# A fused attention and MoE kernel: all four banks of y copied by ScalarE at a tile's end

## The chip, the cores and the metric

The kernel runs on one core of a Trainium2 chip. The time is the device time of one execution in microseconds (us), the median of three runs. Lower is better. The engines are TensorE (PE; PEld is its weight load), VectorE (DVE), ScalarE (ACT), GpSimd (POOL) and SyncE (SP), and they run side by side, ordered by semaphores alone.

## The reference

```python
def _attn_ref(q, k, v, tau):
    qn = q / (np.linalg.norm(q, axis=1, keepdims=True) + 1e-06)
    kn = k / (np.linalg.norm(k, axis=1, keepdims=True) + 1e-06)
    s = kn.transpose(0, 2, 1) @ qn / tau
    s = s - s.max(-1, keepdims=True)
    a = np.exp(s)
    a /= a.sum(-1, keepdims=True) + 1e-09
    return (v @ a).astype(np.float32)

def _moe_ref(x, w_in, w_out, alpha):
    h = x @ w_in
    g = np.maximum(h, 0.0) + alpha * np.minimum(h, 0.0)
    return (g @ w_out).astype(np.float32)
```

q, k and v are 2 x 6016 x 256 in float32, w_in is 256 x 2048 and w_out is 2048 x 256. The attention is over channels, so its matrix a is 256 x 256 for each of the two batches. Its output, as 12032 tokens of 256, goes through the two products with the slope between them.

## The kernel before, in words

For each batch the kernel makes the matrix a, folds it into w_in (the product is called M), and then computes M on v for tiles of tokens. A tile T is two halves of 512 tokens (448 in the last tile of a batch), and there are 12 tiles, six for each batch. The hidden dimension of a tile is worked in 8 groups, so G = 8T + jp runs over 96 groups.

In each group the up-product is done for two blocks of hidden channels and two halves of tokens, with seven block products where eight would be the plain way: sums of blocks of M and of v are multiplied, and the results are combined in the PSUM banks X (`x_ps`), Y (`p_ps`) and Z (`z_ps`). `up` does one block product in three matmuls (high times high, high times low, low times high parts). ScalarE takes X to `h` four times in a group (`take_x`, L747), VectorE adds the banks Y and Z (`add_part`, L1003) and applies the slope (`slope`, L1011), ScalarE rounds `h` to `g_hi` (`split_g_hi`, L757), and VectorE makes `g_lo` from the rest (`split_g_lo`, L1045). `down(G, k)` then multiplies g by w_out in six matmuls (L538) for each of four blocks k, and it is issued one group later than the up-products that it belongs to.

The output of a tile collects in four PSUM banks, `y_ps[t][oc]`, with t the half of tokens and oc the half of output channels. After group 8T + 7's downs, which run among the ups of group 8T + 8, the banks are copied to `y_stage` and stored. Then the next tile may begin to write the same banks: `down(8T + 8, 0)`, issued within group 8T + 9, writes the banks of t = 0, and `down(8T + 8, 1)` those of t = 1. Each waits for the copies of its two banks. There are 11 such boundaries between tiles. At the end of the last tile other code (L876) copies the banks, all on ScalarE.

Before the change ScalarE copies three banks at a boundary: [0][0] at the end of its work for group 8T + 8, and the two of t = 1 in the next group, before and after a `split_g_hi`. VectorE copies [0][1] in `take_y_dve` at the end of its own work for group 8T + 8, ahead of two `split_g_lo`. The order on each engine is the order in which the code issues; nothing reorders it.

Of the kernel before, what the change touches and what calls it, by code (L numbers as in the profile page):

```python
# [5 lines left out]
def build(nc, qk, qk_t, v_t, w_in, w_out, small, y_t):  # L6
# [9 lines left out]
    CC = C // P  # L16
# [4 lines left out]
    FJ = F // P  # L21
# [6 lines left out]
    ALL = B * TILES  # L28
    JP = FJ // 2
    GROUPS = ALL * JP  # L30

    def half_width(T):
        t = T % TILES
        return HALF if t < TILES - 1 else (N - 2 * HALF * (TILES - 1)) // 2

    def first_token(T):
        return T // TILES * N + T % TILES * 2 * HALF
# [41 lines left out]
    with ctx:  # L79
        def sb(name, shape, dt=fp32):  # L80
            return ctx.enter_context(nc.sbuf_tensor(name, shape, dt))

        def pb(name, shape):
            return ctx.enter_context(nc.psum_tensor(name, shape, fp32))

        def sem(name):
            return ctx.enter_context(nc.semaphore(name))
# [56 lines left out]
        y_stage = sb("y_stage", [P, 2, CC, HALF])  # L144
# [14 lines left out]
        y_ps = [[pb(f"y_ps{t}{oc}", [P, HALF]) for oc in range(CC)] for t in range(2)]  # L159
# [22 lines left out]
        y_stored = [sem(f"y_stored{n}") for n in range(2)]  # L182
# [26 lines left out]
        w_lo_ready = sem("w_lo_ready")  # L209
# [21 lines left out]
        down_done = sem("down_done")  # L231
        bank_done = sem("bank_done")
        y_copied = sem("y_copied")
        y_copied_dve = sem("y_copied_dve")
        dve_step = sem("dve_step")


# [38 lines left out]
        def _(sp):  # L276
# [26 lines left out]
            def load_v(T):  # L303
                b, t = T // TILES, T % TILES
                H = half_width(T)
                if T > 0:
# [3 lines left out]
                for kc in range(CC):  # L310
                    sp.dma_start(v_stage[:, 2 * kc:2 * kc + 2, 0:H],
                                 v_t[b, kc, :, n0:n0 + 2 * H].rearrange("p (t h) -> p t h", t=2)
                                 ).then_inc(v_loaded, 16)
# [14 lines left out]
            def store(T, t):  # L328
                H = half_width(T)
                n0 = first_token(T) + t * H  # L330
                sp.wait_ge(y_copied, 3 * T + 1 + 2 * t)
                if t == 0:
                    sp.wait_ge(y_copied_dve, T + 1)
                sp.dma_start(y_v[:, :, n0:n0 + H], y_stage[:, t, :, 0:H]).then_inc(y_stored[t], 16)

            for i in range(RING):
# [52 lines left out]
            H = half_width(ALL - 1)  # L389
            n0 = first_token(ALL - 1)  # L390
            for n in range(2 * CC - 1):
                t, oc = n // CC, n % CC
                sp.wait_ge(y_copied, 3 * (ALL - 1) + n + 1)
                sp.dma_start(y_v[:, oc, n0 + t * H:n0 + (t + 1) * H], y_stage[:, t, oc, 0:H]
                             ).then_inc(y_stored[t], 16)

            sp.wait_ge(y_copied, 3 * (ALL - 1) + 2 * CC)
            sp.dma_start(y_v[:, CC - 1, n0 + H:n0 + H + H // 2], y_stage[:, 1, CC - 1, 0:H // 2]
                         ).then_inc(y_stored[1], 16)
            sp.wait_ge(y_stored[0], 16 * (ALL - 1 + CC))  # L400
# [32 lines left out]
        def _(pe):  # L433
# [84 lines left out]
            def down(G, k):  # L518
                T, jp = G // JP, G % JP
                H = half_width(T)  # L520
                f, t = BLOCKS[k]
                j = 2 * jp + f
                pe.wait_ge(g_lo_ready, 4 * G + k + 1)
                if jp == 0 and k < 2:
                    if T > 0:

                        pe.wait_ge(y_copied, 3 * (T - 1) + 1 + 2 * t)
                        if t == 0:
                            pe.wait_ge(y_copied_dve, T)
                    else:  # L530

                        pe.wait_ge(m_out, CC * (t + 1))
                if T == 0 and k == 0:
                    pe.wait_ge(w_lo_ready, 2 * jp + 2)
                for oc in range(CC):
                    ws = slice(oc * P, (oc + 1) * P)
                    for w_part, g_part in ((w_hi, g_hi), (w_hi, g_lo), (w_lo, g_hi)):
                        product = nc.tensor.matmul(  # L538
                            y_ps[t][oc][:, 0:H], w_part[:, j, ws], g_part[:, k, 0:H],
                            start=jp == 0 and k < 2 and w_part is w_hi and g_part is g_hi,  # L540
                            stop=jp == JP - 1 and k >= 2 and w_part is w_lo, skip_group_check=True)
                product.then_inc(down_done, 1)
# [37 lines left out]
            for G in range(GROUPS):  # L580
                T, jp = G // JP, G % JP
# [64 lines left out]
        def _(act):  # L646
# [38 lines left out]
            def load_exp():  # L685
                nc.scalar.activation(warm[:, :], ones[:, 0:1], ACT.Exp)
# [72 lines left out]
            def take_y(T, t, oc):  # L759
                H = half_width(T)  # L760
                act.wait_ge(down_done, 4 * (JP * T + JP - 1) + 3 + t)
                if T == 0:

                    act.wait_ge(w_lo_ready, FJ)
                else:
                    act.wait_ge(y_stored[t], 16 * T)
                nc.scalar.copy(y_stage[:, t, oc, 0:H], y_ps[t][oc][:, 0:H]).then_inc(y_copied, 1)
# [39 lines left out]
            for G in range(GROUPS):  # L807
                T, jp = G // JP, G % JP
                take_x(G, 0, 0)
                if jp == 1 and T > 0:  # L810
                    take_y(T - 1, 1, 0)
                if G > 0:
                    split_g_hi(G - 1, 3)
                if jp == 1 and T > 0:
                    take_y(T - 1, 1, 1)
                if G == ROOT_G:
                    take_root(1)
                if G == EXP_G:
                    exponentials(1)
                if G == 0:  # L820
                    split_m_hi(0, 1)
                if G == 2:
                    split_m_hi(0, 3)
                if G in M_SPLIT:
                    split_m_hi(*M_SPLIT[G])
                if T + 1 < ALL:
                    for op in (V_ACT_FIRST if T == 0 else V_ACT).get(jp, ()):
                        if T == 0 and op == B11:

                            act.wait_ge(qk1_summed, len(LATE_STEPS))  # L830
                        split_v_hi(T + 1, op)
                take_x(G, 1, 3)
                if G == 0:
                    take_m(0, 2)
                if G in PAIR_AT:
                    split_pair_hi(PAIR_AT[G])
                if G == BROADCAST_G:
                    copy_rq(1)
                if G == MOVE_G:
                    split_at_hi(1)  # L840
                if G in M_AT:
                    take_m(*M_AT[G])
                take_x(G, 2, 1)
                split_g_hi(G, 0)
                if G == 0:
                    split_m_hi(0, 2)
                for n in SQ_AT.get(G, ())[:1]:
                    square_rows(n)
                take_x(G, 3, 2)
                if G == 0:  # L850
                    take_m(0, 3)
                for k in (1, 2) if G < GROUPS - 1 else (2, 1):
                    split_g_hi(G, k)
                if jp == 0 and T > 0:
                    take_y(T - 1, 0, 0)
                for n in SQ_AT.get(G, ())[1:]:
                    square_rows(n)
                if G == SUMS_G:
                    nc.scalar.activation(warm[:, :], ones[:, 0:1], ACT.Sqrt)
                if G == ROOT_G:  # L860
                    load_exp()
                if G in SLICE_AT:
                    split_slice_hi(SLICE_AT[G])
                for j in W_AT.get(G, ()):
                    split_w_hi(j)
            split_g_hi(GROUPS - 1, 3)
            H = half_width(ALL - 1)
            for n in range(2 * CC):
                t, oc = n // CC, n % CC
# [4 lines left out]
                for part in range(parts):  # L874
                    ns = slice(part * H // parts, (part + 1) * H // parts)
                    nc.scalar.copy(y_stage[:, t, oc, ns], y_ps[t][oc][:, ns]).then_inc(y_copied, 1)  # L876
            act.wait_ge(y_copied, 3 * (ALL - 1) + 2 * CC + 1)
            n0 = first_token(ALL - 1) + H
            nc.scalar.dma_start(y_v[:, CC - 1, n0 + H // 2:n0 + H], y_stage[:, 1, CC - 1, H // 2:H]
                                ).then_inc(y_stored[1], 16)  # L880
# [2 lines left out]
        def _(dve):  # L883
# [145 lines left out]
                nc.vector.tensor_tensor(slice_lo[:, :, :], w_slice[:, n % RAW_RING, :, :],  # L1029
                                        slice_hi[:, :, :].bitcast(fp32), ALU.subtract).then_inc(slice_lo_ready, 1)  # L1030

            def take_y_dve(T):
                H = half_width(T)
                dve.wait_ge(down_done, 4 * (JP * T + JP - 1) + 3)
                if T == 0:

                    dve.wait_ge(w_lo_ready, FJ)
                else:
                    dve.wait_ge(y_stored[0], 16 * T)
                nc.vector.tensor_copy(y_stage[:, 0, 1, 0:H], y_ps[0][1][:, 0:H]).then_inc(y_copied_dve, 1)  # L1040

            def split_g_lo(G, k):
                H = half_width(G // JP)
                dve.wait_ge(g_hi_ready, 4 * G + (k + 1 if G < GROUPS - 1 else LAST_ORDER.index(k) + 1))
# [54 lines left out]
            for G in range(GROUPS):  # L1099
                T, jp = G // JP, G % JP  # L1100
# [46 lines left out]
                    split_g_lo(G, 2)  # L1147
                dve.wait_ge(c12_done, G + 1)
                slope(G, 3)
                if jp == 0 and T > 0:  # L1150
                    take_y_dve(T - 1)
                for k in (1, 2) if G < GROUPS - 1 else (1,):
                    split_g_lo(G, k)
                if G == ROOT_G:
# [42 lines left out]
```

## Time and profile before

| | us |
|---|---|
| median of three runs (1076.49 to 1076.99) | 1076.69 |
| time of the profiled execution | 1076.63 |
| its span, first to last instruction | 1074.8 |
| PE busy | 1070.9 |
| PEld busy | 906.2 |
| DVE busy | 847.0 |
| ACT busy | 654.6 |
| POOL busy | 40.4 |

The span and the profiled execution's time differ by what lies around the instructions. Busy time is the union of an engine's instructions; matmuls overlap in it, since one starts before the one ahead has ended. The granted clock of TensorE was 1.0 over the execution.

### The profile page before, as it was taken

How to read it: one execution, taken by the hardware profiler on the slowest of the kernel's cores; microseconds unless marked ns; L12 is line 12 of the kernel's file. 1: busy time of each engine (PE TensorE's matmuls, PEld its weight loads, DVE VectorE, ACT ScalarE, POOL GpSimd, SP SyncE). 2: the span in 40 equal slices, each digit the busy share in tenths (PEclk: the TensorE clock that was granted, in tenths of full speed). 3: DMA queues.
4: the chain of work that ended last, by engine and by line, in shares of the span. 5: the costliest groups of instructions: out<-in, count | busy, mean ns of one | idle time of the engine just before them, and what ended most of it. 6: DMA issues, size and time to landing. Idle time of an engine off the chain costs nothing.

```text
span 1074.8 us, 13902 instructions
## 1 busy us (share of the span) xinstructions
PE 1070.9 (100%) x4995; PEld 906.2 (84%) x4995; DVE 847.0 (79%) x1349; ACT 654.6 (61%) x1100; POOL 40.4 (4%) x54
## 2 busy tenths in 40 slices
PE   9999999999999999999999999999999999999998
PEld 7888888888888888888998888888888888888898
DVE  6999987877877777787798887777777777787776
ACT  6676677667766555655666655555555555555544
POOL 0000000000000000000000000000000000000000
PEclk9999999999999999999999999999999999999999
DMA  9621154455453102103212101201202202200101
GB/s 382 284 88 50 40 158 127 138 160 150 134 162 99 30 13 54 45 9 79 69 30 73 50 11 49 59 8 52 59 1 59 59 0 54 57 1 10 40 1 35
DMA packets 30837, 80.07 MB, mean 74 GB/s; under 512 B 2992, under 2 KB 9264, under 8 KB 29232
## 3 DMA queue, kind: packets, MB, share of 16 engines
q1 hardware_dynamic: 24288, 67.80, 18.1%
q0 software_dynamic: 6336, 11.28, 6.8%
q8 instruction: 39, 0.64, 0.2%
q14 instruction: 30, 0.25, 0.1%
q10 hardware_dynamic: 144, 0.11, 0.0%
HBM read 64.04 MB, written 12.32 MB: 71 GB/s over the span
## 4 chain that ended last, share of the span: by engine, by line
PE 100%; ACT 0%; issue 0%; POOL 0%; POOLq 0%
PE y_ps L538 47%; PE x_ps L512 24%; PE z_ps L512 12%; PE p_ps L512 6%; PE x_ps L444 4%; PE s_ps L464 3%; PE p_ps L498 2%; PE s_ps L444 1%; PE y_ps L498 1%; PE y_ps L553 0%; PE z_ps L440 0%; PE p_ps L486 0%; PE p_ps L473 0%; PE p_ps L479 0%; ACT y_stage L876 0%; PE s_ps L435 0%
## 5 line engine op out<-in xcount | busy, mean ns | idle before, releaser
L538 PE MATMUL y_ps<-g_hi,w_hi 128*128 128x512 f32 (+1 forms) x760 | 293.1, 386 | 0.0
L538 PE MATMUL y_ps<-g_hi,w_lo 128*128 128x512 f32 (+1 forms) x760 | 292.9, 385 | 0.0
L538 PE MATMUL y_ps<-g_lo,w_hi 128*128 128x512 f32 (+1 forms) x760 | 292.9, 385 | 0.0
L757 ACT CAST g_hi<-h 128x512 fp32r<-128x512 f32 (+1 forms) x384 | 234.0, 610 | 78.6 <-DVE h L1011 69.3
L1011 DVE SCALAR_TENSOR_TENSOR h<-h,small_sb 128x512 f32<-128x512 f32 (+1 forms) x384 | 273.7, 733 | 0.0
L1003 DVE SCALAR_TENSOR_TENSOR h<-z_ps,sigma_neg,h 128x512 f32<-128x512 f32 (+1 forms) x192 | 141.7, 738 | 148.0 <-ACT h L747 147.6
L1045 DVE TENSOR_TENSOR g_lo<-h,g_hi 128x512 fp32r<-128x512 f32 (+1 forms) x384 | 249.9, 670 | 0.8 <-ACT g_hi L757 0.5
L747 ACT ACTIVATE h<-x_ps,sigma_neg 128x512 f32<-128x512 f32 (+1 forms) x192 | 130.7, 681 | 175.2 <-PE x_ps L512 165.1
L747 ACT ACTIVATE h<-x_ps,sigma 128x512 f32<-128x512 f32 (+1 forms) x192 | 130.6, 680 | 124.8 <-PE x_ps L512 120.2
L538 PEld LDWEIGHTS y_ps<-g_hi,w_hi 128*128 128x128 f32 x760 | 142.7, 188 | 27.3 <-issue 0.3
L538 PEld LDWEIGHTS y_ps<-g_hi,w_lo 128*128 128x128 f32 x760 | 142.7, 188 | 27.0
L538 PEld LDWEIGHTS y_ps<-g_lo,w_hi 128*128 128x128 f32 x760 | 142.7, 188 | 26.6
L512 PE MATMUL x_ps<-v_hi,m_hi 128*128 128x512 f32 (+1 forms) x384 | 148.8, 388 | 0.0
L512 PE MATMUL x_ps<-v_lo,m_hi 128*128 128x512 f32 (+1 forms) x384 | 148.1, 386 | 0.0
L512 PE MATMUL x_ps<-v_hi,m_lo 128*128 128x512 f32 (+1 forms) x384 | 148.0, 385 | 0.0
L1003 DVE SCALAR_TENSOR_TENSOR h<-p_ps,sigma,h 128x512 f32<-128x512 f32 (+1 forms) x96 | 70.8, 738 | 42.2 <-ACT h L747 42.2
L512 PEld LDWEIGHTS x_ps<-v_hi,m_hi 128*128 128x128 f32 x384 | 72.1, 188 | 14.4 <-ACT h L747 0.9
L512 PEld LDWEIGHTS x_ps<-v_hi,m_lo 128*128 128x128 f32 x384 | 72.1, 188 | 13.6
L512 PEld LDWEIGHTS x_ps<-v_lo,m_hi 128*128 128x128 f32 x384 | 72.1, 188 | 12.9
L512 PE MATMUL z_ps<-v_hi,m_hi 128*128 128x512 f32 (+1 forms) x192 | 74.3, 387 | 0.0
L512 PE MATMUL z_ps<-v_lo,m_hi 128*128 128x512 f32 (+1 forms) x192 | 74.0, 385 | 0.0
L512 PE MATMUL z_ps<-v_hi,m_lo 128*128 128x512 f32 (+1 forms) x192 | 73.9, 385 | 0.0
(129 smaller groups left out, 1009.4 us busy)
## 6 DMA issues: line engine op xcount, KB each, us to landing
rows_t<-qk_t SPq DMA_DIRECT2D x32, 376.0 KB, 4.0
stage<-qk SPq DMA_DIRECT2D x10, 1024.0 KB, 13.3
v_stage<-v_t SPq DMA_DIRECT2D x20, 512.0 KB, 4.6
y_t<-y_stage SPq DMA_DIRECT2D x20, 512.0 KB, 2.8
pair<-qk SPq DMA_DIRECT2D x19, 512.0 KB, 3.7
v_stage<-v_t POOLq DMA_DIRECT2D x27, 256.0 KB, 4.1
scratch<-w_in SPq DMA_DIRECT2D x12, 256.0 KB, 2.8
v_stage<-v_stage POOLq DMA_DIRECT2D x9, 256.0 KB, 3.3
```

Of the source, the lines that this page charges most:

```text
L444: product = nc.tensor.matmul(s_ps[b][:, kc * C:(kc + 1) * C], rows[:, C + kc * P:C + (kc + 1) * P], rows[:, 0:C], start=False, stop=last, ...
L464: product = nc.tensor.matmul(S[:, kc * C:(kc + 1) * C], k_part[:, i, ks], q_part[:, i, 0:C], start=False, stop=n == PAIRS - 1 and i == 1 a ...
L498: product = nc.tensor.matmul(bank[:, kc * 2 * P:(kc + 1) * 2 * P], a_part[:, qc, kc * P:(kc + 1) * P], w_part[:, qc, :], start=a_part is a ...
L512: product = nc.tensor.matmul(bank[:, 0:H], m_part[:, jp, a, :], v_part[T % 2][:, t, 0:H], start=start and m_part is m_hi and v_part is v_h ...
L538: product = nc.tensor.matmul(y_ps[t][oc][:, 0:H], w_part[:, j, ws], g_part[:, k, 0:H], start=jp == 0 and k < 2 and w_part is w_hi and g_pa ...
L747: nc.scalar.mul(h[:, k, 0:H], X[:, 0:H], side(k)[:, j:j + 1]).then_inc(x_copied, 1)
L757: nc.scalar.copy(g_hi[:, k, 0:H], h[:, k, 0:H]).then_inc(g_hi_ready, 1)
L1003: return nc.vector.scalar_tensor_tensor(out=h[:, k, 0:H], in0=bank[:, 0:H], scalar=side(k)[:, j:j + 1], in1=h[:, k, 0:H], op0=ALU.mult, op ...
L1011: nc.vector.scalar_tensor_tensor(out=h[:, k, 0:H], in0=h[:, k, 0:H], scalar=alpha_sb[:, j:j + 1], in1=h[:, k, 0:H], op0=ALU.mult, op1=ALU. ...
L1045: nc.vector.tensor_tensor(g_lo[:, k, 0:H], h[:, k, 0:H], g_hi[:, k, 0:H].bitcast(fp32), ALU.subtract).then_inc(g_lo_ready, 1)
```

## The change

ScalarE gets a fourth copy, of bank [0][1], right behind that of bank [0][0]. `take_y_dve` and its semaphore `y_copied_dve` go. `y_copied` now counts four copies for each tile, and the waits of SP (stores) and of PE (`down` of the next tile) count accordingly.

```diff
@@ store
-                sp.wait_ge(y_copied, 3 * T + 1 + 2 * t)
-                if t == 0:
-                    sp.wait_ge(y_copied_dve, T + 1)
+                sp.wait_ge(y_copied, 4 * T + CC * (t + 1))
@@ down
-                        pe.wait_ge(y_copied, 3 * (T - 1) + 1 + 2 * t)
-                        if t == 0:
-                            pe.wait_ge(y_copied_dve, T)
+                        pe.wait_ge(y_copied, 4 * (T - 1) + CC * (t + 1))
@@ block.scalar
                 if jp == 0 and T > 0:
                     take_y(T - 1, 0, 0)
+                    take_y(T - 1, 0, 1)
...
@@ block.vector
-            def take_y_dve(T):
-                H = half_width(T)
-                dve.wait_ge(down_done, 4 * (JP * T + JP - 1) + 3)
-                if T == 0:
-
-                    dve.wait_ge(w_lo_ready, FJ)
-                else:
-                    dve.wait_ge(y_stored[0], 16 * T)
-                nc.vector.tensor_copy(y_stage[:, 0, 1, 0:H], y_ps[0][1][:, 0:H]).then_inc(y_copied_dve, 1)
...
                 slope(G, 3)
-                if jp == 0 and T > 0:
-                    take_y_dve(T - 1)
                 for k in (1, 2) if G < GROUPS - 1 else (1,):
                     split_g_lo(G, k)
```

The counts at the kernel's end change from 3 to 4 for each tile in the same way, and nothing else there changes.

How ScalarE's instructions stand at the boundary into tile 7 (group 56), before: the last rows of group 56 and the first of group 57.

```order
L757 CAST g_hi<-h 128x512 [waits down_done,g_ready] x2
L767 COPY y_stage<-y_ps 128x512 [waits y_stored0,down_done]
L747 ACTIVATE h<-x_ps,sigma 128x512 [waits g_lo_ready,x_done]
L767 COPY y_stage<-y_ps 128x512 [waits y_stored1,down_done]
L757 CAST g_hi<-h 128x512 [waits down_done,g_ready]
```

And at the same place after the change (ScalarE's lines are numbered five lower from here on):

```order
L752 CAST g_hi<-h 128x512 [waits down_done,g_ready] x2
L762 COPY y_stage<-y_ps 128x512 [waits y_stored0,down_done] x2
L742 ACTIVATE h<-x_ps,sigma 128x512 [waits g_lo_ready,x_done]
L762 COPY y_stage<-y_ps 128x512 [waits y_stored1,down_done]
L752 CAST g_hi<-h 128x512 [waits down_done,g_ready]
```

The one copy has become two, and all that follows in ScalarE's queue stands behind the second.

VectorE's queue at the same boundary, before:

```order
L1003 SCALAR_TENSOR_TENSOR h<-z_ps,sigma_neg,h 128x512 [waits z_done]
L1011 SCALAR_TENSOR_TENSOR h<-h,small_sb 128x512 [waits x_copied]
L1011 SCALAR_TENSOR_TENSOR h<-h,small_sb 128x512 [waits c12_done]
L1040 COPY y_stage<-y_ps 128x512 [waits y_stored0,down_done]
L1045 TENSOR_TENSOR g_lo<-h,g_hi 128x512 [waits g_hi_ready] x2
L1003 SCALAR_TENSOR_TENSOR h<-p_ps,sigma,h 128x512 [waits x_copied,y_done]
L1045 TENSOR_TENSOR g_lo<-h,g_hi 128x512 [waits g_hi_ready]
```

And after (its lines are numbered four lower):

```order
L999 SCALAR_TENSOR_TENSOR h<-z_ps,sigma_neg,h 128x512 [waits z_done]
L1007 SCALAR_TENSOR_TENSOR h<-h,small_sb 128x512 [waits x_copied]
L1007 SCALAR_TENSOR_TENSOR h<-h,small_sb 128x512 [waits c12_done]
L1031 TENSOR_TENSOR g_lo<-h,g_hi 128x512 [waits g_hi_ready] x2
L999 SCALAR_TENSOR_TENSOR h<-p_ps,sigma,h 128x512 [waits x_copied,y_done]
L1031 TENSOR_TENSOR g_lo<-h,g_hi 128x512 [waits g_hi_ready]
```

The copy is gone, and the two subtractions stand directly behind the slope.

## Rows read from the trace of the kernel before

**Rows 1.** The page: busy times and the chain that ended last.
```profile
PE 1070.9 (100%) x4995; PEld 906.2 (84%) x4995; DVE 847.0 (79%) x1349; ACT 654.6 (61%) x1100; POOL 40.4 (4%) x54
...
PE 100%; ACT 0%; issue 0%; POOL 0%; POOLq 0%
```

**Rows 2.** Waits (engine line, released by: us in total, times, longest).
```profile
PEld z_ps L512 <- DVE h L1003: 0.5, 3, 0.2
```

**Rows 3.** Instructions that write y_stage: ns min/median/max, first and last start.
```profile
L767 ACT COPY y_stage<-y_ps x33: 523/578/604, 155.4 to 1005.9; 128x512 f32<-128x512 f32 x30, 128x448 f32<-128x448 f32 x3
...
L1040 DVE COPY y_stage<-y_ps x11: 615/680/683, 155.5 to 1003.6; 128x512 f32<-128x512 f32 x10, 128x448 f32<-128x448 f32 x1
```

**Rows 4.** Timeline, boundary into tile 7: start us, us, engine, instruction [idle before, releaser].
```profile
677.84 0.57 ACT L767 COPY y_stage<-y_ps 128x512 f32<-128x512 f32 x1
677.86 0.68 DVE L1040 COPY y_stage<-y_ps 128x512 f32<-128x512 f32 x1
...
678.58 0.69 ACT L747 ACTIVATE h<-x_ps,sigma 128x512 f32<-128x512 f32 x1 [0.17 <-PE x_ps L512]
...
678.84 0.19 PEld L538 LDWEIGHTS y_ps<-g_hi,w_hi 128*128 128x128 f32 x1
...
680.15 0.60 ACT L767 COPY y_stage<-y_ps 128x512 f32<-128x512 f32 x1
...
680.63 0.64 ACT L659 CAST v_hi<-v_stage 128x512 fp32r<-128x512 f32 x1
...
680.88 0.19 PEld L538 LDWEIGHTS y_ps<-g_hi,w_hi 128*128 128x128 f32 x1
...
681.30 0.69 ACT L747 ACTIVATE h<-x_ps,sigma_neg 128x512 f32<-128x512 f32 x1
...
682.24 0.19 PEld L512 LDWEIGHTS x_ps<-v_hi,m_hi 128*128 128x128 f32 x1
```

**Rows 5.** Timeline, boundary into tile 10, the last of this pattern.
```profile
922.64 0.57 ACT L767 COPY y_stage<-y_ps 128x512 f32<-128x512 f32 x1
...
923.64 0.19 PEld L538 LDWEIGHTS y_ps<-g_hi,w_hi 128*128 128x128 f32 x1
```

**Rows 6.** Timeline, boundary into tile 5, which is 448 wide.
```profile
510.19 0.58 ACT L767 COPY y_stage<-y_ps 128x512 f32<-128x512 f32 x1
...
511.00 0.64 ACT L747 ACTIVATE h<-x_ps,sigma 128x448 f32<-128x448 f32 x1 [0.23 <-PE x_ps L512]
...
511.22 0.19 PEld L538 LDWEIGHTS y_ps<-g_hi,w_hi 128*128 128x128 f32 x1
...
512.47 0.60 ACT L767 COPY y_stage<-y_ps 128x512 f32<-128x512 f32 x1
...
513.04 0.36 PE L512 MATMUL x_ps<-v_hi,m_lo 128*128 128x448 f32 x1
...
513.18 0.19 PEld L538 LDWEIGHTS y_ps<-g_hi,w_hi 128*128 128x128 f32 x1 [0.16 <-issue]
513.24 0.41 PE L538 MATMUL y_ps<-g_hi,w_hi 128*128 128x448 f32 x1
...
513.49 0.36 PE L538 MATMUL y_ps<-g_lo,w_hi 128*128 128x448 f32 x1
```

**Rows 7.** Timeline, boundary into tile 6, whose copies are 448 wide.
```profile
593.46 0.53 ACT L767 COPY y_stage<-y_ps 128x448 f32<-128x448 f32 x1
...
594.27 0.19 PEld L538 LDWEIGHTS y_ps<-g_hi,w_hi 128*128 128x128 f32 x1
```

**Rows 8.** Timeline, boundary into tile 1 (tiles 2 and 3 have the pattern too).
```profile
155.45 0.58 ACT L767 COPY y_stage<-y_ps 128x512 f32<-128x512 f32 x1
...
155.93 0.83 ACT L668 ACTIVATE rows_t<-rows_t 128x752 f32<-128x752 f32 x1
...
157.66 0.69 ACT L747 ACTIVATE h<-x_ps,sigma 128x512 f32<-128x512 f32 x1 [0.81 <-PE x_ps L512]
...
157.91 0.19 PEld L538 LDWEIGHTS y_ps<-g_hi,w_hi 128*128 128x128 f32 x1
```

More of the change, by code:

```diff
@@ L233, in build @@
         y_copied = sem("y_copied")
-        y_copied_dve = sem("y_copied_dve")
         dve_step = sem("dve_step")
@@ L392, in _ @@
                 t, oc = n // CC, n % CC
-                sp.wait_ge(y_copied, 3 * (ALL - 1) + n + 1)
+                sp.wait_ge(y_copied, 4 * (ALL - 1) + n + 1)
                 sp.dma_start(y_v[:, oc, n0 + t * H:n0 + (t + 1) * H], y_stage[:, t, oc, 0:H]
                              ).then_inc(y_stored[t], 16)
-            sp.wait_ge(y_copied, 3 * (ALL - 1) + 2 * CC)
+            sp.wait_ge(y_copied, 4 * (ALL - 1) + 2 * CC)
             sp.dma_start(y_v[:, CC - 1, n0 + H:n0 + H + H // 2], y_stage[:, 1, CC - 1, 0:H // 2]
@@ L876, in _ @@
                     nc.scalar.copy(y_stage[:, t, oc, ns], y_ps[t][oc][:, ns]).then_inc(y_copied, 1)
-            act.wait_ge(y_copied, 3 * (ALL - 1) + 2 * CC + 1)
+            act.wait_ge(y_copied, 4 * (ALL - 1) + 2 * CC + 1)
             n0 = first_token(ALL - 1) + H
```

## Prediction, made before the changed kernel ran

> **What bounds the kernel now.** I read the page first. TensorE is busy for 1070.9 of 1074.8 us, and the chain that ended last is TensorE at 100% [rows 1]. So nothing on VectorE (847.0 us) or ScalarE (654.6 us) is on the path by its length; it counts only where it makes TensorE start something late. The list of waits says how much of that there is: the largest total that VectorE's work holds the weight loads of Z back is 0.5 us in three waits [rows 2]. VectorE relieved of work can thus return almost nothing, and the question is where ScalarE, loaded with more, comes late. Then I read the two copy lines in the instructions that write y_stage [rows 3], and the timeline at each of the 11 boundaries, of which there are four kinds [rows 4 to 8].
>
> In the common kind [rows 4] both engines start to copy within 0.02 us of each other, at 677.84 and 677.86, and the two banks are free at 678.54. The weight load of the next tile's first down comes at 678.84, so both copies were done 0.30 us ahead of it. The bank pair of t = 1 is closer: ScalarE's last copy ends at 680.15 + 0.60 = 680.75, and its weight load comes at 680.88, 0.13 us later. TensorE's order is fixed, and all behind a late load is late.
>
> **What the change does.** It removes 11 copies of 0.68 us from VectorE [rows 3]. Of VectorE's queue the two g_lo subtractions behind the copy, and all up to its next wait, may start up to 0.68 us earlier. TensorE was not waiting for these there, so this is worth 0, with a bound of 0.5 us gained, all that rows 2 give VectorE's hold on Z. On ScalarE it adds 11 copies. A copy there takes 0.58 us (0.53 at 448 columns), but the instruction behind one starts earlier than its end: 0.48 us after its start at 155.45 to 155.93 [rows 8], and again at 680.15 to 680.63 [rows 4]. So I put the second copy 0.48 us after the first, its end at 0.48 + 0.58 = 1.06 us after the first's start, and the instruction after it at 0.96.
>
> How late is late? Rows 6 have the same wait lost once already. The last copy of t = 1 ends at 512.47 + 0.60 = 513.07, and the weight load that waits for it starts at 513.18, so the handover takes 0.11 us. Its matmul ahead started at 513.04, which is when the load would have started, so it is 0.14 late. The matmuls start at 513.04, 513.24 and 513.49: 0.20 and 0.25 us apart where 0.20 is regular, a loss of 0.05. A load that comes late by 0.14 therefore costs 0.05, and I take it that about 0.10 us of lateness is absorbed, and the rest lost for good.
>
> First race, the banks of t = 0. Common kind: 677.84 + 1.06 + 0.11 = 679.01 against 678.84, late by 0.17, a loss of 0.07. Five boundaries are of this kind (into tiles 4, 7, 8, 9 and 10), from copy to load 1.00 us each; the last has 922.64 and 923.64 [rows 5]. 5 x 0.07 = 0.35. Into the 448-wide tiles 5 and 11: 510.19 + 1.17 = 511.36 against 511.22 [rows 6], late by 0.14, a loss of 0.04 each, 0.08. Into tile 6, where the copies are of 448 columns: taking 0.43 as the pace and 0.53 as the length, 593.46 + 0.96 + 0.11 = 594.53 against 594.27 [rows 7], late by 0.26, a loss of 0.16. The three boundaries into tiles 1 to 3 lose nothing: TensorE has other matmuls there, and the load comes 157.91 - 155.45 = 2.46 us after the copy [rows 8]. Sum of the first race: 0.35 + 0.08 + 0.16 = 0.59 us.
>
> Second race, the banks of t = 1. Queued behind the added copy on ScalarE are the first X copy of the next group, the two copies of t = 1 with a g_hi cast between them, a v_hi cast and the next X copy. In the common kind the X copy started at 678.58, when TensorE had released it; now it starts at 677.84 + 0.96 = 678.80, 0.22 later, and the last copy of t = 1 ends at 680.75 + 0.22 = 680.97, with the handover 681.08. The load it holds is itself later by the first race's 0.07, 680.95. Late by 0.13, a loss of 0.03 (x 5 = 0.15). In the 448-wide tiles the X copy moves from 511.00 to 511.15, and the load, which was 0.14 late, becomes 0.14 + 0.15 - 0.04 = 0.25 late: a loss of 0.15 where 0.05 was lost, 0.10 more each, 0.20. Into tile 6 the first race's 0.16 leaves the slack it needs, 0. Sum: 0.35 us.
>
> Third race, the X bank itself. The copy that frees it for the third of its products started at 681.30 and can now start at 681.30 + 0.22 at the latest, to end at 682.21 and be known at 682.32. The weight load that needs it, 682.24, is later by 0.10 from the two races, 682.34. It just holds, so 0; had it failed by 0.1 us it would have been absorbed. The store of t = 0 is issued some 0.4 us later, since its second bank is ready at 678.90 instead of 678.54, but SP's next entry is the store of t = 1, which waited longer before as well. So no other load in SP's queue moves by it, and POOL's are behind VectorE's v_lo, which gets no later. At the kernel's end nothing changes: all copies there were ScalarE's.
>
> Total: 0.59 + 0.35 = 0.94 us more than the profiled 1076.63, 1077.57. The profiled execution is 0.06 below the median of the runs, 1076.69, so I say 1077.6.
>
> What a second copy behind a first takes on ScalarE is not in this trace, so its bounds matter. Below, the handover could be shorter than 0.11 and lateness absorbed whole, if an undisturbed load starts 0.20 us ahead of its matmul (with the matmul before, 513.04, against 513.24 [rows 6]) and needs less than that: no loss at all, 1076.7. Above, the second copy could start only when the first is over, 0.58 instead of 0.48: 0.10 more in both the start and all behind it, on eight boundaries 0.8 in all (it moves the two races alike, and the first's loss then pays for the second's). And if no lateness were absorbed, 16 late loads at 0.10 each would add 1.6 us. I take 0.48, which two rows show.
>
> The Trainium skill's page "ScalarE: Activation LUTs", in its rules for kernel authors, budgets about 0.3 us for each ACTIVATE and 0.83 ns for an element, by estimate 0.72 us for 512 columns. The trace has 0.58 us and a pace of 0.48 [rows 4, 8], so it doesn't agree; by the page's figure the pace of 0.48 would be 0.72, and the sum about 0.24 us more at each of eight boundaries, near 1079.5. The page "TensorEngine Tiling (Array Packing)", under the PSUM bottleneck, says to use both ScalarE and VectorE to empty PSUM, which speaks against this change. Here it is the direction of the two races above.
>
> **Rivals.** (B) All hidden: ScalarE is free enough (654.6 us busy, idle 0.17 us in front of the X copy at 678.58), and the late loads cost nothing because each load precedes its matmul by more than the lateness. For it: the regular loads start when the matmul ahead starts, and 0.10 of 0.14 was absorbed. Against it: 0.05 was lost [rows 6]. Time 1076.7.
>
> (C) Slower: the second copy hands its bank over much later than 1.17 us after the first's start, at all eight boundaries without spare matmuls. The place is the load at 678.84. It decides from 0.27 us of loss for each boundary (8 x 0.27 = 2.16, which is 0.2%), so from a lateness of 0.37, that is a copy that is free 0.20 us later than I reckon. Where copies follow at 0.68, the length of VectorE's [rows 3], it is exactly there. With 0.36 lost for each, 1076.7 + 2.9 = 1079.6. Against it: no ScalarE copy in rows 3 is above 0.604 us.
>
> (D) Faster: VectorE's relief shows. It has 0.5 us at most in rows 2 and at the boundaries nothing to give, unless TensorE's pace itself were better without VectorE reading PSUM beside it. A gain of 0.2% would need 0.2 us at each of 11 boundaries, where the load of 678.84 stands in regular step already. 1074.4.
>
> **How the numbers follow.** (A), my forecast, 1077.6, has 0.60, with its own range 1077.0 to 1078.6; (B) 0.32, (C) 0.06, (D) 0.02. The range from 1076.3 to 1078.8 holds B with the scatter of the runs (0.3 us), A with the bound of 0.8 us on its pace, and leaves out C, D and the far end without absorption. A difference of 0.2% (2.15 us) is about the least that a measurement of this kernel can tell from none, so A and B are both "same": 0.92. Slower is C, 0.06; faster is D, 0.02.
>
> **What would show it.** In the trace after: a second ScalarE copy 0.48 us after the first, at the eight boundaries; the next weight load of y_ps 1.17 us after the first copy's start instead of 1.00, with ScalarE's copy named as what ended its idle time or the matmul interval behind it 0.07 us too long; the X copy behind it at 0.96 with no idle ahead. At the boundaries into tiles 1 to 3 no change of TensorE's. TensorE's span grows by 0.9 us, all of it in these places. I am wrong if the load keeps its 1.00 us (B), if some interval at a boundary grows by 0.3 us or more (C), if losses appear between boundaries, or if the interval between matmuls changes.

## The result and the profile after

The changed kernel took 1078.48 us, the median of 22 runs (1077.91 to 1079.28), and the kernel before 1076.62 (22 runs, 1076.24 to 1077.41). The ratio is 1.0018 with a 95% interval of 1.0012 to 1.0024: 1.86 us slower, inside the stated range and short of the 0.2% taken as the least that can be told, but clear of zero and twice the 0.94 us forecast.

The head of the page of the changed kernel answers to [rows 1]. TensorE is still the whole chain, and its busy time has grown by 2.3 us. VectorE has lost 4.9 us and ScalarE gained 4.0.

```profile
span 1077.1 us, 13891 instructions
...
PE 1073.2 (100%) x4995; PEld 905.9 (84%) x4995; DVE 842.1 (78%) x1338; ACT 658.6 (61%) x1111; POOL 40.4 (4%) x54
...
q14 instruction: 30, 0.25, 0.1%
...
PE 100%; ACT 0%; issue 0%; POOL 0%; POOLq 0%
```

The instructions that write y_stage answer to [rows 3]: 44 ScalarE copies, the longest 0.617 us where it was 0.604.

```profile
L762 ACT COPY y_stage<-y_ps x44: 526/590/617, 155.7 to 1007.9; 128x512 f32<-128x512 f32 x40, 128x448 f32<-128x448 f32 x4
```

The timeline of the boundary into tile 7 answers to [rows 4].

```profile
679.03 1.06 ACT L762 COPY y_stage<-y_ps 128x512 f32<-128x512 f32 x2
...
679.98 0.70 ACT L742 ACTIVATE h<-x_ps,sigma 128x512 f32<-128x512 f32 x1
...
680.20 0.19 PEld L533 LDWEIGHTS y_ps<-g_hi,w_hi 128*128 128x128 f32 x1 [0.21 <-issue]
680.25 0.46 PE L533 MATMUL y_ps<-g_hi,w_hi 128*128 128x512 f32 x1
680.55 0.39 PE L533 MATMUL y_ps<-g_lo,w_hi 128*128 128x512 f32 x1
...
680.77 0.39 PE L533 MATMUL y_ps<-g_hi,w_lo 128*128 128x512 f32 x1
...
682.27 0.19 PEld L533 LDWEIGHTS y_ps<-g_hi,w_hi 128*128 128x128 f32 x1 [0.15 <-issue]
```

The two copies end 1.06 us after the first's start, as forecast, and the next instruction of ScalarE starts at 0.95 (0.96 forecast). The weight load comes at 680.20, 1.17 us after 679.03, where it came 1.00 after before. Its matmul starts at 680.25, the one behind at 680.55 and the next at 680.77: one interval of 0.30 where 0.22 to 0.23 is regular. The second weight load (682.27) waits again. Both waits read "issue": the view names no releaser for them, and the timeline has to be read beside it.

The waits of TensorE's weight loads show where else it comes late; the row on Z answers to [rows 2].

```profile
PEld y_ps L533 <- issue: 2.3, 12, 0.2
...
PEld z_ps L509 <- DVE h L999: 1.1, 5, 0.4
PEld y_ps L533 <- DVE g_lo L1031: 0.7, 3, 0.3
```

To see what each place costs I compared the starts of TensorE's 4995 matmuls in the two traces, one by one. The distance between the traces grows only in a few places:

| place | growth, us |
|---|---|
| before 66 us | 0.23 |
| boundaries into tiles 1 to 3 | 0.00 |
| boundaries into tiles 4, 7, 8, 9, 10 | 5 x 0.107 (0.09 at the first race, 0.017 at the second) |
| boundary into tile 5 | 0.07 + 0.13 |
| boundary into tile 6 | 0.17 + 0.03 |
| boundary into tile 11 | 0.09 + 0.08 |
| one place at 632.5 | 0.19 to 0.21 |
| one place at 819.3 | 0.24 |
| inside the 448-wide tiles 5 and 11, behind their boundaries | 0.27 + 0.17 |

The eight boundaries make 1.11 us; of this up to 0.1 may be scatter, since the kernel before against itself grows by 0.05 at each of the boundaries into tiles 5 and 11. The two single places make 0.45, and nothing in the forecast speaks of them. The traces of the other kernels differ by -0.6 to +0.5 us already before 66 us, in whichever kernel, so that row is an execution's own scatter.

At the second of the single places VectorE starts late. In the kernel before:

```profile
815.94 0.69 ACT L747 ACTIVATE h<-x_ps,sigma_neg 128x512 f32<-128x512 f32 x1 [1.35 <-PE x_ps L512]
...
816.74 0.75 DVE L1003 SCALAR_TENSOR_TENSOR h<-z_ps,sigma_neg,h 128x512 f32<-128x512 f32 x1 [2.15 <-ACT h L747]
...
817.78 0.39 PE L512 MATMUL z_ps<-v_hi,m_hi 128*128 128x512 f32 x1
```

And the same instructions in the changed kernel:

```profile
817.35 0.69 ACT L742 ACTIVATE h<-x_ps,sigma_neg 128x512 f32<-128x512 f32 x1 [1.35 <-PE x_ps L509]
...
818.49 0.75 DVE L999 SCALAR_TENSOR_TENSOR h<-z_ps,sigma_neg,h 128x512 f32<-128x512 f32 x1 [2.50 <-ACT h L742]
...
819.29 0.50 PE L509 MATMUL z_ps<-v_hi,m_hi 128*128 128x512 f32 x1
```

ScalarE's copy of X ends at 816.63 before and 818.04 after. VectorE, idle for over 2 us in both, starts 0.10 us behind it before and 0.45 after. TensorE's load of Z waits for that addition; it comes 0.33 us late and costs 0.24. Of all traces' VectorE starts behind the head, the changed kernel has two such late ones, of 0.15 us at 630.3 and of 0.45 at 818.5, the kernel before none.

The other one leads to the place at 632.5. In the kernel before the weight load of X there was already 0.11 us behind its usual place (its matmul ahead started at 631.21), which cost nothing:

```profile
631.21 0.39 PE L538 MATMUL y_ps<-g_hi,w_lo 128*128 128x512 f32 x1
631.32 0.19 PEld L512 LDWEIGHTS x_ps<-v_hi,m_hi 128*128 128x128 f32 x1
```

In the changed kernel VectorE's addition starts late, ScalarE's X copy behind it too, and this load is another 0.19 us late:

```profile
630.32 0.75 DVE L999 SCALAR_TENSOR_TENSOR h<-p_ps,sigma,h 128x512 f32<-128x512 f32 x1 [0.15 <-issue]
...
632.50 0.19 PEld L509 LDWEIGHTS x_ps<-v_hi,m_hi 128*128 128x128 f32 x1 [0.33 <-ACT h L742]
```

It costs 0.17 to 0.19, all of what was added: what can be absorbed was used up before.

### The profile page after: what moved, and what is told of

Same layout as the page of the kernel before. It is cut to its first block, busy times and chain, and to the rows that moved or that the text cites. A ratio compares the mean times of both kernels' runs of the same rounds, so it can differ in the third digit from the quotient of the medians.

```text
span 1077.1 us, 13891 instructions
## 1 busy us (share of the span) xinstructions
PE 1073.2 (100%) x4995; PEld 905.9 (84%) x4995; DVE 842.1 (78%) x1338; ACT 658.6 (61%) x1111; POOL 40.4 (4%) x54
## 4 chain that ended last, share of the span: by engine, by line
PE 100%; ACT 0%; issue 0%; POOL 0%; POOLq 0%
PE y_ps L533 47%; PE x_ps L509 24%; PE z_ps L509 12%; PE p_ps L509 6%; PE x_ps L441 4%; PE s_ps L461 3%; PE p_ps L495 2%; PE s_ps L441 1%; PE y_ps L495 1%; PE y_ps L548 0%; PE z_ps L437 0%; PE p_ps L483 0%; PE p_ps L470 0%; PE p_ps L476 0%; ACT y_stage L872 0%; PE s_ps L432 0%
```

## Experiments

Each kernel was timed against the kernel before on the same chip. With 11 runs of each kernel (4 of the doubled copy) beside 21 to 33 of the kernel before, a ratio's interval is about 0.0009 to either side, 1 us, so differences of half a microsecond rest on the traces. "Growth" is again the distance of TensorE's matmul starts from the first trace of the kernel before.

| kernel | median us | before | ratio (95%) | boundaries, growth us | the two late VectorE starts |
|---|---|---|---|---|---|
| changed, again | 1078.65 | 1076.74 | 1.0018 (1.0009 to 1.0027) | 1.15 | yes |
| VectorE's part alone | 1077.42 | 1076.74 | 1.0004 (0.9995 to 1.0013) | 0.01 | yes |
| ScalarE's part alone | 1077.84 | 1076.74 | 1.0012 (1.0003 to 1.0021) | 1.08 | no |
| early copies | 1077.09 | 1076.74 | 1.0003 (0.9994 to 1.0012) | -0.01 | yes |
| changed, with ticks | 1078.16 | 1076.87 | 1.0011 (1.0003 to 1.0020) | 1.10 | no |
| copied twice | 1082.30 | 1076.87 | 1.0051 (1.0036 to 1.0067) | 5.17 | yes |
| second race alone | 1077.84 | 1076.87 | 1.0011 (1.0002 to 1.0020) | 1.09 | no |
| before, again | 1076.99 | 1076.87 | 1.0003 (0.9994 to 1.0012) | 0.07 | no |
| early copies, with ticks | 1076.82 | 1077.01 | 1.0001 (0.9992 to 1.0010) | -0.02 | no |
| all four early, with ticks | 1077.51 | 1077.01 | 1.0006 (0.9997 to 1.0015) | 0.26 | no |

### The changed kernel again

No edit.

> The changed kernel once more, unchanged. In its first trace TensorE lost 1.11 us at the eight boundaries (0.107 at each of the common kind, 0.20, 0.20 and 0.17 at the others) and about 0.7 us elsewhere: one stall of 0.19 at 632.5, one of 0.22 at 819.3, the rest in the 448-wide tiles. Theory A (late handover of the banks by ScalarE's queue): the boundary losses come again to within 0.01 us, since they follow from the order alone, and the time is again 1.0018 of the kernel before. If what lies elsewhere is chance of one execution, it stands in other places now; if the change causes it (theory R: the moved instructions of VectorE and ScalarE), the sum elsewhere is again 0.5 to 0.9 us.

The same ratio. The boundary losses came again, 0.09 at the first race of tiles 7 to 9; into tiles 4 and 10 0.06 and then about 0.07 at the second race, so not all to within 0.01 us. The two single places are there again, at 632.0 (0.19) and 818.8 (0.25), at the same instructions: not chance. Inside tile 5 the growth was 0.54 instead of 0.27, inside tile 11 -0.01 instead of 0.17: these do vary.

### VectorE's part alone

```diff
-                if jp == 0 and T > 0:
-                    take_y_dve(T - 1)
...
-                        if t == 0:
-                            pe.wait_ge(y_copied_dve, T)
```

Nobody copies bank [0][1] of the first 11 tiles here.

> VectorE's part alone: its copy of bank [0][1] is gone and nobody makes it in its place (this bank is not copied for the tiles but the last), and ScalarE's queue is as before. Theory A: VectorE's relief is worth nothing and costs nothing, TensorE's boundaries are as before, 1076.6 us, within 0.3 us of the kernel before. Theory R: VectorE's earlier subtractions cause the 0.7 us outside the boundaries, 1077.2 to 1077.4. A gain by relief would show as 1076.1 or less.

No loss at the boundaries, but both single places, 0.17 and 0.25 us, and the time 0.7 us above the kernel before by the medians (the ratio's interval holds 1). So to free VectorE of the copy has a price, 0.42 us by the trace, and it isn't the load on any engine.

### ScalarE's part alone

```diff
                 if jp == 0 and T > 0:
                     take_y(T - 1, 0, 0)
+                    take_again(T - 1, 0, 0)
```

`take_again` copies the bank into a spare bf16 tile and counts in `y_copied`; `take_y_dve` stays.

> ScalarE's part alone: VectorE keeps its copy of bank [0][1], and ScalarE copies bank [0][0] twice, the second time into a spare bf16 tile; TensorE waits for both and for VectorE's. Theory A: the same losses as in the changed kernel at all eight boundaries (0.09 at the first race and 0.02 at the second of the common kind), 1.1 us there, and if all of the change's cost is ScalarE's, 1078.5 us. Theory R (VectorE's shift causes what lies elsewhere): 1077.7.

1.08 us at the boundaries, neither single place. 1.1 us above the kernel before by the medians: near the 1077.7 of theory R, and against the 1078.5 of "all is ScalarE's". The two parts, 1.1 and 0.7, come near the 1.9 of the change, though with 1 us of uncertainty on each this sum shows little; the traces carry the division.

In this kernel the first weight load came 1.13 us after the first copy (678.31 to 679.44) instead of 1.17, since it started 0.07 us behind the second copy's end where the changed kernel has 0.11, and cost 0.03 to 0.05, and the second race cost more, 0.07 to 0.09. A longer loss at the first race shields the second.

### The copies of t = 0 moved earlier

```diff
                 for k in (1, 2) if G < GROUPS - 1 else (2, 1):
                     split_g_hi(G, k)
-                if jp == 0 and T > 0:
-                    take_y(T - 1, 0, 0)
-                    take_y(T - 1, 0, 1)
+                    if jp == 0 and T > 0:
+                        take_y(T - 1, 0, k - 1)
```

> The changed kernel with the copies of t = 0 moved earlier in ScalarE's queue: bank [0][0] between the casts of g_hi of blocks 1 and 2, where ScalarE was idle for 0.70 us, and bank [0][1] behind the second cast, where the first copy stood. Theory A: TensorE's loads at the boundaries come as in the kernel before (1.00 us after the last copy's start), the 1.1 us are gone, and the time is 1076.6, no more than 0.3 us from the kernel before. Theory R: what lies outside the boundaries stays, 1077.2 to 1077.4.

ScalarE's timeline at the boundary into tile 7:

```profile
675.75 0.62 ACT L752 CAST g_hi<-h 128x512 fp32r<-128x512 f32 x1
...
676.28 0.58 ACT L762 COPY y_stage<-y_ps 128x512 f32<-128x512 f32 x1
...
677.08 0.62 ACT L752 CAST g_hi<-h 128x512 fp32r<-128x512 f32 x1 [0.22 <-DVE h L1006]
677.60 0.58 ACT L762 COPY y_stage<-y_ps 128x512 f32<-128x512 f32 x1
678.35 0.69 ACT L742 ACTIVATE h<-x_ps,sigma 128x512 f32<-128x512 f32 x1 [0.17 <-PE x_ps L509]
678.61 0.19 PEld L533 LDWEIGHTS y_ps<-g_hi,w_hi 128*128 128x128 f32 x1
```

One copy fits in the 0.70 us of idle time, the second stands where the only one stood, and the load comes 1.01 us after it without a wait. The growth at the boundaries is gone (-0.01 us), the two single places stay (0.18 and 0.25). That the boundary losses come from ScalarE's order is shown; the copies themselves, 44 as in the changed kernel, cost TensorE nothing there.

### The changed kernel with ticks

```diff
+            def tick(T):
+                dve.wait_ge(down_done, 4 * (JP * T + JP - 1) + 3)
+                if T == 0:
+                    dve.wait_ge(w_lo_ready, FJ)
+                else:
+                    dve.wait_ge(y_stored[0], 16 * T)
+                nc.vector.tensor_copy(mark[:, T:T + 1], ones[:, 0:1])
...
                 slope(G, 3)
+                if jp == 0 and T > 0:
+                    tick(T - 1)
```

> The changed kernel with 11 tiny VectorE copies (128x1, into a spare tile that nobody reads) where the copies of bank [0][1] stood, with the same waits ahead. ScalarE's queue is that of the changed kernel. The traces of the changed kernel (both) and of the two kernels whose VectorE lost its copy have the same two late VectorE starts, 0.15 us at 630.3 and 0.45 us at 818.5, at VectorE's instructions 959 and 1215, which are 256 apart; no kernel whose VectorE kept the copy has them. Theory I (a VectorE instruction at certain positions of its stream starts late, and taking 22 entries out of the stream moved two sensitive ones there): with the count restored both vanish, TensorE's stalls at 632.5 and 819.3 too (0.19 and 0.24 us), and the time is that of ScalarE's part alone, 1077.8. Theory R2 (it is the freed 0.68 us of VectorE that moves the phase): both stay, 1078.5.

Both late starts are gone. The same two instructions here:

```profile
816.84 0.69 ACT L743 ACTIVATE h<-x_ps,sigma_neg 128x512 f32<-128x512 f32 x1 [1.35 <-PE x_ps L510]
...
817.63 0.75 DVE L1000 SCALAR_TENSOR_TENSOR h<-z_ps,sigma_neg,h 128x512 f32<-128x512 f32 x1 [2.15 <-ACT h L743]
```

Again 0.10 us from ScalarE's end to VectorE's start, and TensorE's stalls at both places are gone. A tick is 0.15 us of work where the copy was 0.68, and yet both late starts go: it is not VectorE's time that counts, but the entries in its queue. Counted from VectorE's first entry in the trace, which is number 0, waits included, the late starts are at numbers 959 and 1215, 256 apart, in all five traces that have them, though they stand at 628.9 to 631.8 and 816.8 to 821.0 us. The kernel before has 1587 entries, the changed one 1565: 11 copies and 11 waits fewer. The change moved an addition of a bank, one that TensorE waits for, to number 1215, where a v_lo subtraction stood that nobody was waiting for. In the kernel before the instructions at both numbers follow straight on a busy one, with no idle time ahead. No run shifted the count by another number of entries, so which shifts hurt was not tried. The time, 1078.16, lies between the two expectations (1077.8 and 1078.5), and decides nothing alone.

The Trainium skill, "Runtime: NRT & Kernel Launch", on instruction fetch mechanics, says that an engine's instructions are refilled in blocks of 256 and that the crossing is mostly hidden. The distance of 256 agrees with it. "Mostly hidden" does too for numbers 447, 703 and 1471, where no late start is seen; at 959 and 1215 it was 0.15 and 0.45 us.

The traces say more. The profile's page has 30 packets of instructions on queue 14, each of 8192 bytes, and in every one of the twelve traces such packets stand at about every 128th entry of VectorE's, so twice as often as blocks of 256 would ask. One stands at 959 or 960 and one between 1213 and 1218, and they move with the count: from 624.0 and 802.9 us in the kernel before to 629.5 and 818.8 with VectorE's part alone, where ScalarE's queue is unchanged, and with the ticks to 624.9 and 803.8. So both late starts lie where instructions are being loaded. That the loading makes them late is not shown: the packets near them start 0.7 and 1.7 us after the late instruction (631.0 and 820.2 in the changed kernel), and those of the other kernels bring no late start.

### Bank [0][1] copied twice

```diff
                     take_y(T - 1, 0, 1)
+                    take_again(T - 1, 0, 1)
...
-                        pe.wait_ge(y_copied, 4 * (T - 1) + CC * (t + 1))
+                        pe.wait_ge(y_copied, 5 * (T - 1) + 3 + CC * t)
```

> The changed kernel with bank [0][1] copied by ScalarE a second time, into a spare bf16 tile, right behind, and TensorE waits for all three copies. Theory A (a late weight load costs its lateness less 0.10 us): the load of the common kind comes 1.65 us after the first copy's start instead of 1.00, late by 0.65, and costs 0.55; 0.52 in the 448-wide tiles and 0.59 into tile 6, 4.4 in all, with 0.3 from the second race and 0.7 as in the changed kernel elsewhere: 1082.0 us. Rival (the loss is in proportion, half of the lateness): 0.33 for each, 2.6 us, with the rest 1080.2.

```profile
680.50 1.06 ACT L763 COPY y_stage<-y_ps 128x512 f32<-128x512 f32 x2
...
681.44 0.60 ACT L770 CAST spare<-y_ps 128x512 bf16<-128x512 f32 x1
...
682.16 0.19 PEld L534 LDWEIGHTS y_ps<-g_hi,w_hi 128*128 128x128 f32 x1 [0.70 <-DVE g_lo L1040]
682.19 0.47 PE L534 MATMUL y_ps<-g_hi,w_hi 128*128 128x512 f32 x1 [0.31 <-ACT spare L770]
```

The load comes 1.66 us after the first copy (1.65 expected), late by 0.66, and costs 0.57, the same to 0.001 us at seven of the eight boundaries. Late by 0.17 to 0.18 costs 0.09, late by 0.66 costs 0.57. So 0.09 us is absorbed and the rest lost one for one; the proportional rival (0.33) is out. The load of Z at 819.3 in the changed kernel, late by 0.33 for 0.24, lies between and agrees. The time, 1082.3, is 5.4 us above the kernel before, 5.1 expected. The releaser named at the load, g_lo, is wrong here: it had been done; the one named at the matmul is right.

### The second race alone

```diff
                 if jp == 0 and T > 0:
                     take_y(T - 1, 0, 0)
+                    take_again(T - 1, 1, 0)
...
-                        pe.wait_ge(y_copied, 3 * (T - 1) + 1 + 2 * t)
+                        pe.wait_ge(y_copied, 4 * (T - 1) + 1 + 3 * t)
```

> The second race alone: the kernel before, VectorE's copy included, with one more ScalarE copy behind that of bank [0][0], of bank [1][0] into a spare bf16 tile, for which only the down of t = 1 waits. Theory A: the first load at a boundary comes as in the kernel before; the second is late by 0.20 in the common kind and costs 0.10, 0.14 more than before in the 448-wide tiles and 0.09 into tile 6, 0.9 us in all: 1077.6. None of the two late VectorE starts, since its count is that of the kernel before. Rival (all loss is at the first race, and what follows is hidden): 1076.7.

```profile
677.93 0.58 ACT L768 COPY y_stage<-y_ps 128x512 f32<-128x512 f32 x1
678.41 0.59 ACT L775 CAST spare<-y_ps 128x512 bf16<-128x512 f32 x1
678.89 0.70 ACT L748 ACTIVATE h<-x_ps,sigma 128x512 f32<-128x512 f32 x1
678.93 0.19 PEld L539 LDWEIGHTS y_ps<-g_hi,w_hi 128*128 128x128 f32 x1
...
680.45 0.61 ACT L768 COPY y_stage<-y_ps 128x512 f32<-128x512 f32 x1
...
681.18 0.19 PEld L539 LDWEIGHTS y_ps<-g_hi,w_hi 128*128 128x128 f32 x1 [0.24 <-issue]
```

The first load keeps its 1.00 us, the second is late by 0.21 and costs 0.12 to 0.13: 1.09 us in all, 0.9 expected, and the time is 1.0 above. The copy was not one that TensorE waited for at the first load, yet it costs as much, because what stands behind it in ScalarE's queue is handed over later. VectorE's count was that of the kernel before, and no late start came.

### The kernel before again

> The kernel before once more, unchanged, for the scatter of a trace and of a time: 1.0000 of itself within 0.0005, TensorE's step at every boundary the same to 0.01 us, and the 448-wide tiles (510 to 593 and from 1004 on), where the traces so far differ by -0.2 to +0.7 us, different from the first trace by some tenths if they are chance.

The growth is 0.00 us at eight of the eleven boundaries, -0.02 at one and 0.05 at the two into the 448-wide tiles. Inside these tiles it is 0.12 and 0.52 us: in the same kernel, so it belongs to the execution. In each group there the load of Z waits 0.13 to 0.17 us for an addition of VectorE's, and goes from the one value to the other.

### Early copies with ticks

The edits of the early copies and of the ticks together.

> Both cures at once: all four copies on ScalarE with the two of t = 0 moved earlier in its queue, and the 11 tiny VectorE copies that keep the positions of its instructions. Theory (handover and position together explain the change): boundaries as in the kernel before, no stall at 631 and 818, 1076.8 us, within 0.3 us of the kernel before. If something else of the change costs time, 1077.1 or more stays, as in the kernel with the early copies alone.

The growth is -0.02 us at the boundaries and none at the single places, and the median is 1076.82 beside 1077.01 for the kernel before. With both cures, all four copies on ScalarE cost nothing that can be measured, but gain nothing either.

### All four early

```diff
+                if jp == 1 and T > 0:
+                    take_y(T - 1, 1, 1)
                 if G > 0:
                     split_g_hi(G - 1, 3)
-                if jp == 1 and T > 0:
-                    take_y(T - 1, 1, 1)
```

> The same with the last copy of t = 1 ahead of the g_hi cast instead of behind it, so that all four copies are early. Theory: the 0.05 us that the kernel before lost at each of the boundaries into the 448-wide tiles (513.2 and 1006.6) vanish too, since the banks of t = 1 are free 0.5 us sooner; 0.1 us in all, which the time can't tell, 1076.7. A cost would show if the g_hi cast, half a microsecond later, held back VectorE's g_lo and with it the down of block 3: 0.1 us or more at each boundary.

The small gain did not come, the cost did, and at other places than before: 0.11 to 0.14 us in each of tiles 1 to 3 and at the boundaries into tiles 5 and 11. At the boundary into tile 5:

```profile
511.90 1.07 ACT L763 COPY y_stage<-y_ps 128x512 f32<-128x512 f32 x2
...
512.85 0.59 ACT L753 CAST g_hi<-h 128x448 fp32r<-128x448 f32 x1
...
513.47 0.63 DVE L1039 TENSOR_TENSOR g_lo<-h,g_hi 128x448 fp32r<-128x448 f32 x1 [0.67 <-ACT g_hi L753]
...
514.19 0.64 ACT L743 ACTIVATE h<-x_ps,sigma_neg 128x448 f32<-128x448 f32 x1 [0.23 <-DVE g_lo L1039]
...
514.87 0.19 PEld L510 LDWEIGHTS x_ps<-v_hi,m_hi 128*128 128x128 f32 x1 [0.27 <-ACT h L743]
```

The cast of g_hi comes 0.5 us later, VectorE idles 0.67 us for it, ScalarE's X copy waits for that g_lo to free its part of h, and TensorE's load of X is late by 0.25. The expectation named the down of block 3 as what would be held back; it was the X bank. Where the g_hi cast stood was already right.

## Why the prediction was right or wrong

**The bound and the direction: right.** TensorE stays the whole chain, slower by less than 0.2% was the likeliest, and the time lies in the range. In part that is luck: the range reached up to 1078.8 for a slower pace of the second copy, which did not come, and what filled it was a loss that the prediction had at nothing. The boundaries alone would have given 1077.7 (1076.62 + 1.11), and the kernel with ScalarE's part alone took 1077.84. One of the prediction's own signs of being wrong, losses between boundaries, did appear. And 0.2% was too coarse for what a time can tell: with 22 runs of each the interval is 0.06% to either side.

**Pace and handover: right.** The second copy ends at 1.06 us and the load comes at 1.17, both as worked out, at the common boundaries. The trace of the kernel before was enough for this.

**First race: right, somewhat low.** 0.59 us was forecast and 0.78 measured: 0.09 instead of 0.07 in the common kind, 0.07 and 0.09 instead of 0.04 in the 448-wide tiles, 0.17 instead of 0.16 into tile 6. Absorption is 0.09 us (0.66 late, 0.57 lost), not quite the 0.10 taken from one place.

**Second race: right in sum, with errors that cancel.** 0.35 forecast, 0.33 measured (5 x 0.017, 0.13, 0.03, 0.08). In the common kind the load was late by 0.11 instead of 0.13 and cost 0.017 instead of 0.03; the two boundaries into 448-wide tiles hold up to 0.05 of scatter each. The experiment that has it alone shows that it isn't an addition to the first but stands behind it: alone it costs 1.09.

**Tiles 1 to 3, third race, the kernel's end: right**, 0.00 us of growth at each of these three boundaries.

**The 0.72 us for a ScalarE copy was not for this case.** The row of the Trainium skill's page "ScalarE: Activation LUTs" from which the prediction worked out 0.72 us is for an ACTIVATE whose bias is a pointer operand; the plain copy has none, so its 0.58 us neither bears the page out nor contradicts it. ScalarE's X copies, which read a factor (sigma) for each partition, took 0.69. The 1079.5 us worked out from it was no forecast for these copies.

**The step that failed is the one on VectorE's relief**: "TensorE was not waiting for these there, so this is worth 0, with a bound of 0.5 us gained". It had no loss in its bounds, and it was a loss of 0.45 us (0.42 in the kernel with VectorE's part alone). Removing the copy took 22 entries out of VectorE's queue, and two instructions that TensorE depends on came to stand at numbers 959 and 1215 of it, where they start late. VectorE's part alone has the losses with no boundary loss, ScalarE's part alone the reverse, and the ticks remove them. That work taken away can't cost holds for the work, and not for the position of what follows it.

**What is not accounted for.** 1.11 + 0.45 = 1.56 of 1.86 us. The remaining 0.3 fits the 448-wide tiles, where the two traces of the changed kernel grew by 0.44 and 0.53, but the kernel before against itself grew by 0.64 there and the kernel with early copies shrank by 0.2, so no trace can say whether the change has a part in it. It stays open.

**Rivals.** B (hidden) fell: the load does not keep its 1.00 us. C asked for 0.27 us of loss at a boundary, and the largest was 0.21. D (relief shows as a gain) fell, with the sign turned round.

## What to carry to other kernels

When the bounding engine never idles, the value of moving work between the others is set by the few handovers with little slack: take the release time from the timeline, add the handover, and count what exceeds the small part that is absorbed. An engine that is 61% busy can still be the wrong place for 0.5 us, and the same work 1.3 us earlier in its queue, in a gap that was there, costs nothing. A change that only removes instructions can still cost, since it moves all later ones; compare a late start in the trace with the instruction's number in its queue, and with the times of the instruction packets, before blaming the work.

## What the runs showed of the hardware

- A VectorE instruction at certain positions of its stream started 0.15 and 0.45 us late, at numbers 959 and 1215 of the trace's count in five traces out of five with the shortened stream, and not where the count was restored by 11 copies of 128x1. Packets of instructions (8192 bytes, queue 14) stand at about every 128th entry of VectorE's in all twelve traces, these two numbers among them. Whether they cause the late start was not tried.
- A weight load that came late by 0.17 to 0.18 us cost TensorE 0.09, late by 0.33 cost 0.24, late by 0.66 cost 0.57, and late by 0.11 cost 0.02: about 0.09 us is absorbed. A load that is on time starts 0.22 us ahead of its own matmul (median of the kernel before); why no more than 0.09 of that is spare was not tried.
- Two ScalarE copies of 128x512 from PSUM back to back took 1.06 us, the instruction behind started 0.48 us after the second. From a ScalarE copy's end to a weight load waiting for it took 0.11 us, and 0.07 in the kernel with ScalarE's part alone.
